# Heads' rows through DRAM, filler products on TensorE, and a new order in the first chunks and short slots

## The chip, the cores and the metric

One core of a Trainium2 chip runs the whole program. The metric is the device time of one execution in microseconds. Three runs of the kernel before gave 1003.18, 1003.45 and 1007.49 us; the median is 1003.45 us.

## The reference

A complex linear recurrence runs over 4 batches, 8 heads, 768 steps and a head width of 48; two layers of a gated network follow on its 3072 tokens.

```python
mag = np.sqrt(a_re * a_re + a_im * a_im)
scale = np.minimum(mag, 0.999) / (mag + 1e-06)           # a is scaled to this length
for t in range(S):                                       # S = 768, per batch and head, state 48 x 48
    new_re = ar * S_re - ai * S_im                       # ar, ai: [:, :, t, :, None]
    new_im = ar * S_im + ai * S_re
    S_re, S_im = new_re + einsum('bhd,bhe->bhde', k[:, :, t], v[:, :, t]), new_im
    y[:, :, t] = einsum('bhd,bhde->bhe', q[:, :, t], S_re)
x = y as (3072, 384)                                     # tokens x (heads * width)
h = x @ w_in;  x = (h * clip(h + 3, 0, 6) / 6) @ w_out              # w_in 384 x 2048
h = x @ w2_in; out = (max(h, 0) + alpha * min(h, 0)) @ w2_out
```

## The kernel before, in words

The recurrence is done in 24 chunks of 128 steps, six to a batch. For one chunk the Scalar engine (ACT) and the Vector engine (DVE) work out, from `a`, the length and angle of each step (`squares`, `logs`, `inverses`, `angle` on ACT; `mags`, `residue`, `refine`, `ratio`, `decays` on DVE), the running products and angles (`forward`, `phases`, `fractions`, `backward` on DVE), cosine and sine (`waves` on ACT), and from these the turned queries and keys (`with_qk`, `product(c, 0)`, `product(c, 1)` on DVE). The products lie in `prod` with 128 rows: rows 0 to 95 hold heads 0 to 5 in pairs, rows 96 to 127 hold the two last heads, 32 rows of their 96 in each of three columns. TensorE wants real and imaginary rows of a head stacked in 96 rows, in `st`. `stack(c)` on SyncE's queue (SP) moves them there by 12 small transfers within the on-chip memory: for each of the two products two for heads 0 to 5 (`low_stack`) and four for the last heads (`high_stack`). Where `two_queues(c)` holds (the first chunks and those made in a short slot), ACT's queue issues two of the twelve.

TensorE then makes a chunk's scores (`score`, two halves), turns its keys (`turn_k`, copied by ACT's `copy_k`), and after DVE's `mask` the outputs (`outputs`) and the new state (`new_state`, added by DVE's `state`). ACT's `x_high` and DVE's `x_low` split the outputs into a high and a low part for the layers.

The first layer runs in ten units: six of 256 columns, four of 384; the second in six units of 512. A unit has 16 items, one for each 128 of the 2048 hidden columns. Item `n` has a `hidden` product (three passes of high and low parts; one 32-bit pass in unit 0), a gate (`gate_of` on ACT, `gate1` on DVE), the split of the gated columns (`high` on ACT, `low` on GpSimd), and an `output` product. TensorE runs `hidden` three items ahead, ACT and DVE the gate two items ahead. At a unit's end ACT's `leave` empties the accumulators. ACT's and DVE's `split_w` split the first layer's weights into high and low parts, 24 blocks, one an item from item 3 on.

The order is written out by hand. `SHORT` and `LONG` cut one chunk's steps into letters, and `places()` deals them over the items of a slot: slot `s` (5 to 8 items, given by `LENGTHS`) holds TensorE's work on chunk `c0 = s`, the second half of the preparation of `c1 = s + 1`, and the first half of `c2 = s + 2`. Slots 2 to 14 are short (`is_short`: units of 256 columns), the others long. Each engine has its own loop over `places()` and runs its steps in the order of its loop; a step that waits holds all behind it on that engine. In a short slot the items' letters are `a`, `cf`, `deos`, `glv`, `hi`, `j`, `kb`. The first two chunks come ahead of item 0, in an order of their own on each engine.

In a slot's first item ACT runs `gate_of`, `copy_k(c0, 0)`, `waves(c1)`, then `high`; in its second `gate_of`, `copy_k(c0, 1)`, `logs(c2)` with a table load, `high`, `copy_ends(c1)`, the weight split and, at a unit's end, `leave`. DVE runs `phases(c1)` and `fractions(c1)` ahead of the first item's `gate1`, and `mask` behind `backward` in the second. In the third item DVE runs `gate1`, `with_qk(c1)` and `product(c1, 0)`, in the fourth `gate1` and `product(c1, 1)`. SP runs `stack(c1)` in the fourth item, `load_qk(c2)` behind it, `load_v(c1)` in the sixth and `load_a(c0 + 4)` in the last. `score(c1, 0)` waits for all twelve transfers.

Of the kernel before, what the change touches and what calls it, by code (L numbers as in the profile page):

```python
# [7 lines left out]
F32 = mybir.dt.float32  # L8
# [45 lines left out]

HIGH_PARTS = [(96, 32, 0, 6, 0), (96, 16, 1, 6, 32), (112, 16, 1, 7, 0), (96, 32, 2, 7, 16)]
STACK_DMAS = 2 * (2 + len(HIGH_PARTS))

# [20 lines left out]
B_BLOCKS = [(1, n) for n in range(NWI)]  # L78
W_ORDER = [b for q in range(NQ) for b in A_BLOCKS[q] + B_BLOCKS[(0, 1, 3, 6)[q]:(1, 3, 6, NWI)[q]]]

W_ITEM = 3
NRP = 12
# [51 lines left out]

def two_queues(c):

    return c <= FIRST or is_short(c - 1)


def splits_at(n):  # L140

    return range(max(0, n - W_ITEM), min(max(0, n + 1 - W_ITEM), len(W_ORDER)))

# [63 lines left out]
def build(nc, a_in, qk_in, v_in, w1_in, w1_out, w2_in, w2_out, alpha, x2_dram, out):  # L207
    with ExitStack() as ctx:
# [73 lines left out]
        guard = raw[0:ROWS2, 0:GUARD * 2 * PAIRS * CH].rearrange("p (c x t) -> p c x t", c=GUARD, x=2)  # L282

        hp = ctx.enter_context(nc.psum_tensor("hp", [P, 2, 512], F32))
        op = ctx.enter_context(nc.psum_tensor("op", [P, KT_DM, 512], F32))
# [9 lines left out]
        a_landed = [sem(f"a_landed{i}") for i in range(2)]  # L295
        st_landed = [sem(f"st_landed{i}") for i in range(2)]
        qk_landed, v_landed = sem("qk_landed"), sem("v_landed")
        wa_landed = [sem(f"wa_landed{i}") for i in range(10)]
# [56 lines left out]

        def high_stack(c, x):
            return [(st[x * HD + d0:x * HD + d0 + rows, c % 2, h, :, :].rearrange("p q t -> p (q t)"),
                     prod[p0:p0 + rows, x, k, :, :].rearrange("p q t -> p (q t)")) for p0, rows, k, h, d0 in HIGH_PARTS]

# [33 lines left out]
        def _(sp):  # L393
# [69 lines left out]
            load_qk(1)  # L463
            stack(0)
            load_a(3)
            load_w(7)
            stack(1)
            load_qk(2)
            load_v(1)
            for k in range(KT_DM):  # L470
                load_w(2 * k + 1)
            load_a(4)
            stack(2)
            load_w(8)
            load_w(9)
# [5 lines left out]
            for steps, n, c0, c1, c2, c3 in places():  # L481
                if "g" in steps:
                    if c1 is not None:
                        stack(c1)
                    if c2 is not None:
                        load_qk(c2)
                if "j" in steps and c1 is not None:
# [101 lines left out]
        def _(act):  # L589
# [3 lines left out]

            def logs(c):
                if c > 0:
# [26 lines left out]
            def copy_ends(c):  # L622
                act.wait_ge(end_step, 2 * c + 1)

                if c > 0:
                    act.wait_ge(st_landed[(c - 1) % 2], 16 * STACK_DMAS * ((c - 1) // 2 + 1))
                act.activation(prod[:, :, :, 0, CH], end_floor[:, c, :].unsqueeze(1).to_broadcast([P, 2, KT_DM]),
                               ACT.Copy).then_inc(ends_set, 1)

            def waves(c):  # L630
# [6 lines left out]
                               ).then_inc(trig_set, 1)  # L637

            def stack(c):
                act.wait_ge(ends_set, c + 1)  # L640
                act.wait_ge(prod_done, 2 * c + 2)
                for to, rows in low_stack(c, 1):
                    act.dma_start(to, rows).then_inc(st_landed[c % 2], 16)

# [69 lines left out]
            squares(2)  # L714
            stack(0)
            waves(1)
            copy_ends(1)
            logs(2)
            copy_k(0, 0)
            stack(1)  # L720
            inverses(2)
            copy_k(0, 1)
            x_high(0)
            angle(2)
            squares(3)
            copy_ends(2)
            copy_k(1, 0)
            waves(2)
            copy_k(1, 1)
            logs(3)  # L730
            x_high(1)
            inverses(3)
            stack(2)
            gate_of(0)
            gate_of(1)
            squares(4)
            for n in range(ALONE):
                gate_of(n + GSTEP)
                if n == 0:
                    angle(3)  # L740

            for steps, n, c0, c1, c2, c3 in places():
                keeps = not is_last(c0)
                gate_of(n + GSTEP)
                if "a" in steps:
                    if keeps:
                        copy_k(c0, 0)
                    if c1 is not None:
                        waves(c1)
                if "c" in steps:  # L750
                    if keeps:
                        copy_k(c0, 1)
                    if c2 is not None:
                        logs(c2)
                if "s" in steps and c3 is not None:
# [3 lines left out]
                if "h" in steps:  # L759
                    x_high(c0)  # L760
                    if c1 is not None and two_queues(c1):
                        stack(c1)
                if "k" in steps and c2 is not None:
                    angle(c2)
                if n + GSTEP >= MT_FF:
                    high(n + GSTEP)
                if "c" in steps and c1 is not None:
                    copy_ends(c1)
                for w in splits_at(n):
                    split_w(w)  # L770
                if n % MT_FF == MT_FF - 1:
                    leave(n // MT_FF)
            for n in range(N1 - MT_FF, NT):
# [39 lines left out]
        def _(dve):  # L813
# [69 lines left out]
            def product(c, x):  # L883
                dve.wait_ge(trig_set, c + 1)

                if c > 0:
                    dve.wait_ge(st_landed[(c - 1) % 2], 16 * STACK_DMAS * ((c - 1) // 2 + 1))
                dve.wait_ge(qb_done, c + 1)
# [125 lines left out]
            forward(1)  # L1014
            backward(1)
            phases(1)
            fractions(1)
            with_qk(1)
            mags(2)
            product(1, 0)  # L1020
# [4 lines left out]
            decay_parts(2)  # L1025
            forward(2)
            backward(2)
            phases(2)
            mask(1, 0)
            fractions(2)  # L1030
            state(0)
            mask(1, 1)
            with_qk(2)
            mags(3)
            product(2, 0)
            product(2, 1)
            residue(3)
            refine(3)
            ratio(3)
            gate1(0)  # L1040
            decays(3)
            gate1(1)
            state(1)
# [3 lines left out]
            for n in range(1, ALONE):  # L1047
                gate1(n + GSTEP)

            for steps, n, c0, c1, c2, c3 in places():  # L1050
# [10 lines left out]
                if "e" in steps and c1 is not None:  # L1061
                    product(c1, 0)
                if "f" in steps:
                    mask(c0, 0)
# [155 lines left out]
        def _(pe):  # L1220
            def score(c, k):
                if k == 0:
                    pe.wait_ge(st_landed[c % 2], 16 * STACK_DMAS * (c // 2 + 1))
                    if c >= FIRST:
# [107 lines left out]

            for c in range(FIRST):
                for k in range(2):
                    score(c, k)
                    turn_k(c, k)
                outputs(c)
                if c < FIRST - 1:
                    new_state(c)
            hidden(0)  # L1340
# [84 lines left out]
```

## Time and profile before

| | us |
|---|---|
| median of the runs | 1003.45 |
| the profiled execution | 1005.47 |
| its span | 1003.8 |
| TensorE busy | 961.2 (96%) |
| weight loads busy | 864.6 |
| DVE busy | 583.0 (58%) |
| ACT busy | 502.1 (50%) |
| GpSimd busy | 269.9 (27%) |

The profile is one execution. An engine's busy time is the sum over its instructions; the waits say which engine or transfer ended an engine's idle time; the chain of waits follows the work that ended last back from its end. Matmul ends are modelled, so a busy TensorE may still run slowly: the length of like instructions at different times tells more.

### The profile page before, as it was taken

The page shows a single profiled execution, that of the slowest core. Times are in us where ns is not written, and L with a number is a line of the kernel's source. Part 1 is how long each engine was busy: PE and PEld are TensorE (multiplying, and loading weights), DVE is VectorE, ACT ScalarE, POOL GpSimd, SP SyncE. Part 2 cuts the span into 40 slices and gives each one's busy share as a digit, 9 for nine tenths or more (in the row PEclk, how much of TensorE's full clock was granted, in tenths as well). Part 3 has the DMA queues.
Part 4 walks back from the last instruction along what each step waited for, and adds up shares of the span by engine and source line. Part 5 has one row for each costly group of instructions (what it writes and reads, how often), then busy time and mean ns, then how long its engine had stood idle before and what let it go on. Part 6 is the DMA issues. An engine that isn't in the chain of part 4 may idle for free.

```text
span 1003.8 us, 17714 instructions
## 1 busy us (share of the span) xinstructions
PE 961.2 (96%) x6786; PEld 864.6 (86%) x6786; DVE 583.0 (58%) x1049; ACT 502.1 (50%) x907; POOL 269.9 (27%) x251
## 2 busy tenths in 40 slices
PE   0899988999999999999999999999999999999998
PEld 0788988899999999999999998888888888888786
DVE  6767886867777767777662345444434444344332
ACT  7766877667877777776643443322222222222211
POOL 0000222222333322322222333332333333323232
PEclk9999999999999999999999999999999999999999
DMA  7753333332333332333320801023060060230000
GB/s 206 202 131 80 96 75 97 93 101 73 88 96 101 97 98 72 95 88 81 82 70 2 306 1 56 1 72 87 0 153 6 1 157 1 72 86 1 32 1 32
DMA packets 83589, 79.97 MB, mean 80 GB/s; under 512 B 32688, under 2 KB 78256, under 8 KB 83120
## 3 DMA queue, kind: packets, MB, share of 16 engines
q1 hardware_dynamic: 78384, 74.07, 27.7%
q10 hardware_dynamic: 5120, 4.76, 1.9%
q8 instruction: 54, 0.88, 0.4%
q14 instruction: 31, 0.25, 0.1%
HBM read 50.34 MB, written 9.44 MB: 60 GB/s over the span
## 4 chain that ended last, share of the span: by engine, by line
PE 85%; DVE 5%; ACT 3%; issue 2%; SPq 2%; DMA 1%; ACTq 0%; DVEq 0%
PE op L1262 12%; PE hp L1263 12%; PE op L1263 12%; PE hp L1262 12%; PE op L1264 12%; PE hp L1264 12%; PE yp L1250 3%; PE gp L1257 2%; PE hp L1285 2%; PE gp L1229 2%; PE yp L1229 2%; PE op L1310 2%; SPq L437 1%; PE tp L1238 1%; DMA st<-prod 1%
## 5 line engine op out<-in xcount | busy, mean ns | idle before, releaser
L572 POOL TENSOR_TENSOR g_lo<-gated,g_hi 128x512 fp32r<-128x512 f32 (+2 forms) x240 | 267.7, 1116 | 726.0 <-ACT g_hi L673 726.0
L673 ACT ACTIVATE g_hi<-gated 128x512 fp32r<-128x512 f32 (+2 forms) x240 | 126.3, 526 | 320.7 <-DVE gated L968 273.7
L964 DVE TENSOR_SCALAR gate<-hp,alpha_sb 128x512 f32<-128x512 f32 x96 | 72.0, 750 | 209.4 <-PE hp L1264 209.4
L953 DVE SCALAR_TENSOR_TENSOR gated<-gate,hp 128x256 f32<-128x256 f32 (+1 forms) x160 | 75.2, 470 | 134.2 <-ACT gate L666 133.8
L1262 PE MATMUL op<-g_hi,wb_hi 128*128 128x256 f32 (+1 forms) x432 | 137.3, 318 | 3.3 <-ACT out_sb L678 2.0
L1262 PE MATMUL hp<-x_hi,wa_hi 128*128 128x256 f32 (+1 forms) x432 | 134.7, 312 | 1.8 <-DVE gated L953 1.5
L1264 PE MATMUL op<-g_hi,wb_lo 128*128 128x256 f32 (+1 forms) x432 | 132.5, 307 | 0.0
L1263 PE MATMUL op<-g_lo,wb_hi 128*128 128x256 f32 (+1 forms) x432 | 132.3, 306 | 0.0
L1264 PE MATMUL hp<-x_hi,wa_lo 128*128 128x256 f32 (+1 forms) x432 | 132.2, 306 | 0.0
L1263 PE MATMUL hp<-x_lo,wa_hi 128*128 128x256 f32 (+1 forms) x432 | 132.2, 306 | 0.0
L666 ACT ACTIVATE gate<-hp,half 128x256 f32<-128x256 f32 (+1 forms) x160 | 81.1, 507 | 93.1 <-PE hp L1264 80.9
L1263 PE MATMUL hp<-x_lo,w2i_hi 128*128 128x512 f32 x288 | 114.6, 398 | 0.0
L1263 PE MATMUL op<-g_lo,wa_hi 128*128 128x512 f32 x288 | 113.8, 395 | 0.0
L1262 PE MATMUL hp<-x_hi,w2i_hi 128*128 128x512 f32 x288 | 113.6, 395 | 0.0
L1262 PE MATMUL op<-g_hi,wa_hi 128*128 128x512 f32 x288 | 113.6, 394 | 0.0
L1264 PE MATMUL hp<-x_hi,w2i_lo 128*128 128x512 f32 x288 | 112.9, 392 | 0.0
L1264 PE MATMUL op<-g_hi,wa_lo 128*128 128x512 f32 x288 | 112.8, 392 | 0.0
L1262 PEld LDWEIGHTS op<-g_hi,wb_hi 128*128 128x128 f32 x432 | 82.1, 190 | 5.1 <-ACT out_sb L678 2.2
L1262 PEld LDWEIGHTS hp<-x_hi,wa_hi 128*128 128x128 f32 x432 | 82.2, 190 | 2.6 <-issue 1.9
L1263 PEld LDWEIGHTS op<-g_lo,wb_hi 128*128 128x128 f32 x432 | 82.2, 190 | 0.1
L1263 PEld LDWEIGHTS hp<-x_lo,wa_hi 128*128 128x128 f32 x432 | 82.1, 190 | 0.1
L1264 PEld LDWEIGHTS op<-g_hi,wb_lo 128*128 128x128 f32 x432 | 82.1, 190 | 0.0
(113 smaller groups left out, 1645.9 us busy)
## 6 DMA issues: line engine op xcount, KB each, us to landing
st<-prod SPq DMA_DIRECT2D x64, 145.1 KB, 3.1
raw<-a_in SPq DMA_DIRECT2D x4, 2304.0 KB, 15.1
a_sb<-a_in SPq DMA_DIRECT2D x24, 288.0 KB, 3.9
qk_sb<-qk_in SPq DMA_DIRECT2D x24, 288.0 KB, 3.5
st<-prod ACTq DMA_DIRECT2D x32, 145.1 KB, 2.6
v_pad<-v_in SPq DMA_DIRECT2D x24, 192.0 KB, 3.6
x_raw<-x SPq DMA_DIRECT2D x6, 768.0 KB, 16.2
out<-out_sb SPq DMA_DIRECT2D x5, 768.0 KB, 4.2
```

The costliest lines, as they stand in the source:

```text
L572: pool.tensor_tensor(g_lo[:, at, 0:wide], gated[:, at * UT:at * UT + wide], g_hi[:, at, 0:wide].bitcast(F32), ALU.subtract).then_inc(glo_d ...
L666: act.activation(gate[:, n % 2 * UT:n % 2 * UT + wide], hp[:, n % 2, 0:wide], ACT.Relu, bias=half[:, 0:1], scale=1.0 / 6.0).then_inc(gate_ ...
L673: act.activation(g_hi[:, at, 0:wide], gated[:, at * UT:at * UT + wide], ACT.Copy).then_inc(ghi_done, 1)
L953: dve.scalar_tensor_tensor(out=gated[:, to], in0=gate[:, at], scalar=1.0, in1=hp[:, n % 2, 0:wide], op0=ALU.min, op1=ALU.mult).then_inc(ga ...
L964: dve.tensor_scalar(gate[:, at], hp[:, n % 2, 0:wide], 0.0, alpha_sb[:, m:m + 1], ALU.min, ALU.mult).then_inc(gate_done, 1)
L1229: mm = pe.matmul(score_banks[k][:, h % G4, :], st[:, c % 2, h, 1, 0:CH], st[:, c % 2, h, 0, 0:CH], start=True, stop=True)
L1250: mm = pe.matmul(y_place(c)[q * BAND:(q + 1) * BAND, j, :], weights, st[:, c % 2, h, 0, 0:CH] if of_state else scores[:, h, :], start=firs ...
L1257: mm = pe.matmul(kv_place(c)[:, h, :], k_rows[:, h, :], v_pad[:, h * PADW:h * PADW + HD], start=True, stop=True)
L1262: pe.matmul(acc, lhs[0], rhs[0], start=start, stop=False)
L1263: pe.matmul(acc, lhs[0], rhs[1], start=False, stop=False)
L1264: return pe.matmul(acc, lhs[1], rhs[0], start=False, stop=stop)
L1285: mm = pe.matmul(hp[:, n % 2, 0:wide], wa_raw[:, at], x_raw[:, u, k, 0:wide], start=k == 0, stop=k == KT_DM - 1)
```

## The change

`high_stack` goes. The 32 rows of the last two heads go out to a DRAM buffer, `rows_dram`, with one transfer for each product (`high_out`) and come back into `st` with one more each (`high_in`), which SP issues in a new step `stack_high` once the first has landed. A chunk's stack is then 8 transfers, all of SP's queue; ACT's `stack` and `two_queues` go. In a slot SP issues `load_qk(c2)` between `stack(c1)` and `stack_high(c1)`.

TensorE gets `busy(count)`: products of a tile of ones with itself into an unused bank, 36 of them among the first two chunks' steps, the first 20 as soon as `product(0, 1)` is done.

On ACT and DVE the order of the first three chunks' steps is written anew. In short slots ACT runs `high`, the weight splits and `leave` straight behind `gate_of` and `copy_k` and ahead of `waves`, `logs`, `squares`, `inverses` and `angle` (the table load of `logs` goes ahead of `high`), and DVE runs `gate1` ahead of `phases` and `fractions`, and `mask` ahead of `backward`. The weight splits follow a plan, `SPLIT_PLAN`: one or two an item from item 1 on, so that the last comes in item 16 (it was item 26).

```diff
-W_ORDER = [b for q in range(NQ) for b in A_BLOCKS[q] + B_BLOCKS[...]]
-W_ITEM = 3
+def usable(block):
+    return -(-(block[1] + 1) * WPC // DM) if block[0] else block[2] * WPC // P + 1
+def split_plan():
+    left = [b for q in range(NQ) for b in A_BLOCKS[q]] + B_BLOCKS
+    plan = {}
+    for n in range(1, 2 * MT_FF):
+        plan[n] = [b for b in left if usable(b) <= n][:1 + n % 2]
+        left = [b for b in left if b not in plan[n]]
...
+        def high_out(x):
+            return (rows_dram[x].rearrange("(k i) f -> i k f", i=HIGH),
+                    prod[LOW:P, x, :, :, :].rearrange("p k q t -> p k (q t)"))
+        def high_in(c, x):
+            return (st[x * HD:x * HD + HD, c % 2, 6:HEADS, :, :].rearrange("p h q t -> p h (q t)"),
+                    rows_dram[x].rearrange("(h d) f -> d h f", d=HD))
...
 # SP, stack(c)
-                sp.wait_ge(prod_done, 2 * c + 1)
-                for to, rows in low_stack(c, 0) + high_stack(c, 0):
-                    sp.dma_start(to, rows).then_inc(st_landed[c % 2], 16)
-                sp.wait_ge(prod_done, 2 * c + 2)
-                for to, rows in high_stack(c, 1) + ([] if two_queues(c) else low_stack(c, 1)):
+                for x in range(2):
+                    sp.wait_ge(prod_done, 2 * c + x + 1)
+                    to, rows = high_out(x)
+                    sp.dma_start(to, rows).then_inc(rows_out[x], 16)
+                    for to, rows in low_stack(c, x):
+                        sp.dma_start(to, rows).then_inc(st_landed[c % 2], 16)
+            def stack_high(c):
+                for x in range(2):
+                    sp.wait_ge(rows_out[x], 16 * (c + 1))
+                    to, rows = high_in(c, x)
                     sp.dma_start(to, rows).then_inc(st_landed[c % 2], 16)
...
 # ACT, a slot's item
+                if "a" in steps and keeps:
+                    copy_k(c0, 0)
+                if "c" in steps and keeps:
+                    copy_k(c0, 1)
+                if is_short(c0):
+                    if "c" in steps and c2 is not None:
+                        act.preload_act_table_set("natural_log_exp_and_others")
+                    behind_gate(n)                 # high(n + GSTEP), split_w, leave
+                    if "c" in steps and c1 is not None:
+                        copy_ends(c1)
+                if "a" in steps and c1 is not None:
+                    waves(c1)
+                if "c" in steps and c2 is not None:
+                    logs(c2, is_short(c0))
...
 # DVE, a slot's item
+                if is_short(c0):
+                    gate1(n + GSTEP)
                 if "a" in steps and c1 is not None:
                     phases(c1)
                     fractions(c1)
-                gate1(n + GSTEP)
+                if not is_short(c0):
+                    gate1(n + GSTEP)
+                elif "f" in steps:
+                    mask(c0, 0)
+                    mask(c0, 1)
...
 # TensorE, the first chunks
+            def busy(count):
+                for _ in range(count):
+                    pe.matmul(hp[:, 1, 0:CH], ones[:, :], ones[:, :], start=True, stop=True)
+            pe.wait_ge(consts_set, 2)
+            pe.wait_ge(prod_done, 2)
+            busy(20)
+            score(0, 0)
+            turn_k(0, 0)
+            score(0, 1)
+            busy(4)
+            turn_k(0, 1)
+            busy(3)
+            outputs(0)
+            busy(3)
+            new_state(0)
+            busy(6)
+            score(1, 0)
+            score(1, 1)
+            turn_k(1, 0)
+            outputs(1)
+            turn_k(1, 1)
```

## Rows read from the trace of the kernel before

**Rows 1.** Busy time by stretch; columns: stretch, length, each engine's busy time, clock, DMA.

```profile
26.94:47.26 20.32, 18.49 (x161) 16.63 (x161) 15.28 (x29) 15.45 (x28) 0.00 (x0) 1.00 0.82 228
47.26:98.33 51.07, 51.07 (x399) 45.46 (x400) 36.45 (x77) 34.86 (x65) 0.00 (x0) 1.00 0.42 104
98.33:203.39 105.06, 95.96 (x940) 91.81 (x939) 82.90 (x165) 77.69 (x157) 26.70 (x31) 0.98 0.36 92
203.39:1003.80 800.41, 795.69 (x5291) 710.70 (x5290) 429.74 (x733) 355.35 (x630) 241.04 (x209) 1.00 0.26 69
199.98:203.39 3.41, 3.41 (x18) 3.41 (x18) 0.83 (x2) 2.24 (x5) 0.72 (x1) 0.50 0.54 143
```

**Rows 2.** TensorE's waits from 98.33 to 203.39: total us, times, longest.

```profile
PE gp L1229 <- DMA st<-prod: 2.4, 3, 1.6
PE op L1262 <- ACT out_sb L678: 2.0, 1, 2.0
PE yp L1250 <- DVE scores L911: 1.6, 2, 0.8
PE hp L1262 <- DVE gated L953: 1.5, 1, 1.5
PE op L1262 <- POOL g_lo L572: 1.3, 3, 0.9
```

**Rows 3.** TensorE in order of time, score products of four chunks: start, length.

```profile
26.94 2.08 PE L1229 MATMUL gp<-st 96*128 96x128 f32 x8 [26.94 <-DMA st<-prod]
...
60.50 1.06 PE L1229 MATMUL gp<-st 96*128 96x128 f32 x8
...
221.17 1.06 PE L1229 MATMUL gp<-st 96*128 96x128 f32 x8
...
242.21 1.05 PE L1229 MATMUL gp<-st 96*128 96x128 f32 x8
```

**Rows 4.** The chain of waits, from chunk 1's last transfer to its outputs.

```profile
35.32 2.48 DMA st<-prod
...
43.11 3.58 PE op L1250 x64
```

**Rows 5.** The chain of waits in slot 7: start, length, what.

```profile
182.29 1.28 ACT L596
...
187.21 1.28 DVE prod L889
...
194.51 3.92 DMA st<-prod
```

**Rows 6.** ACT in order of time, last item of slot 8, first of slot 9.

```profile
219.70 1.28 ACT L616 ACT_TABLE_LOAD   x1
...
221.98 0.40 ACT L673 ACTIVATE g_hi<-gated 128x256 fp32r<-128x256 f32 x1
222.29 0.45 ACT L666 ACTIVATE gate<-hp,half 128x256 f32<-128x256 f32 x1
```

**Rows 7.** DVE in order of time, same place and slot 9.

```profile
219.93 0.41 DVE L953 SCALAR_TENSOR_TENSOR gated<-gate,hp 128x256 f32<-128x256 f32 x1
...
222.23 1.67 DVE L845 TENSOR_TENSOR_SCAN t_phase<-ones,t_frac,t_dt 128x128 f32<-128x128 f32 x3
...
232.35 1.27 DVE L889 TENSOR_TENSOR prod<-t_fb,t_trig 128x768 f32<-128x768 f32 x1
```

**Rows 8.** SP's issues in slot 9: start, time to issue, lines, transfers.

```profile
233.71 4.10 SPq L437 DMA_DIRECT2D st<-prod  x6
237.85 2.48 SPq L440 DMA_DIRECT2D st<-prod  x4
240.38 0.61 SPq L399 DMA_DIRECT2D qk_sb<-qk_in  x1
241.03 1.07 SPq L403 DMA_DIRECT2D qk_sb<-qk_in  x2
```

**Rows 9.** Transfers by size over the span: KB each, median us from issue to landing.

```profile
st<-prod SPq DMA_DIRECT2D x64, 145.1 KB, 3.1
...
x<-out_sb SPq DMA_DIRECT2D x2, 192.0 KB, 3.5
```

**Rows 10.** DVE's weight splits by form: busy, mean ns.

```profile
L905 DVE TENSOR_TENSOR wb_lo<-wb_raw,wb_hi 128x512 fp32r<-128x512 f32 x12 | 8.6, 717 | 6.4 <-ACT wb_hi L683 6.4
```

More of the change, by code:

```diff
@@ L53 @@
 TW = CH + 1
[L55 to L56 removed]
+ROWS_DMAS = 2 * 3
 N1 = U1 * MT_FF
@@ L78 @@
 B_BLOCKS = [(1, n) for n in range(NWI)]
-W_ORDER = [b for q in range(NQ) for b in A_BLOCKS[q] + B_BLOCKS[(0, 1, 3, 6)[q]:(1, 3, 6, NWI)[q]]]
-W_ITEM = 3
+def usable(block):
[6 more added lines that the diff above has]
+        left = [b for b in left if b not in plan[n]]
+    assert not left
+    return plan
+SPLIT_PLAN = split_plan()
+W_ORDER = [b for n in SPLIT_PLAN for b in SPLIT_PLAN[n]]
 NRP = 12
@@ L132, in is_short @@
     return width(items_of(s)[-1] // MT_FF) == FIRST * CH
-def two_queues(c):
-    return c <= FIRST or is_short(c - 1)
 def splits_at(n):
-    return range(max(0, n - W_ITEM), min(max(0, n + 1 - W_ITEM), len(W_ORDER)))
+    return [W_ORDER.index(b) for b in SPLIT_PLAN.get(n, [])]
 def split_count(blocks):
@@ L282, in build @@
         guard = raw[0:ROWS2, 0:GUARD * 2 * PAIRS * CH].rearrange("p (c x t) -> p c x t", c=GUARD, x=2)
+        rows_dram = nc.dram_tensor("rows", (2, LOW, 2 * TW), F32, kind="Internal").ap()
         hp = ctx.enter_context(nc.psum_tensor("hp", [P, 2, 512], F32))
@@ L296, in build @@
         st_landed = [sem(f"st_landed{i}") for i in range(2)]
+        rows_out = [sem(f"rows_out{i}") for i in range(2)]
         qk_landed, v_landed = sem("qk_landed"), sem("v_landed")
@@ L486, in _ @@
                         load_qk(c2)
+                    if c1 is not None:
+                        stack_high(c1)
                 if "j" in steps and c1 is not None:
@@ L592, in squares, with logs @@
                 act.activation(t_sq[:, :, :, :], a_sb[:, c % 2, :, :, :], ACT.Square).then_inc(squares_set, 1)
-            def logs(c):
-                if c > 0:
+            def logs(c, loaded=False):
+                if c > 0 and not loaded:
                     act.preload_act_table_set("natural_log_exp_and_others")
@@ L637, in waves @@
                                ).then_inc(trig_set, 1)
[L639 to L643, printed above, removed]
             def copy_k(c, k):
@@ L719, in _, with behind_gate @@
             copy_k(0, 0)
-            stack(1)
             inverses(2)
+            x_high(0)
             copy_k(0, 1)
-            x_high(0)
             angle(2)
             squares(3)
+            waves(2)
+            copy_k(1, 0)
             copy_ends(2)
-            copy_k(1, 0)
-            waves(2)
+            x_high(1)
             copy_k(1, 1)
             logs(3)
-            x_high(1)
+            gate_of(0)
             inverses(3)
-            stack(2)
-            gate_of(0)
             gate_of(1)
             squares(4)
+            def behind_gate(n):
+                if n + GSTEP >= MT_FF:
+                    high(n + GSTEP)
+                for w in splits_at(n):
+                    split_w(w)
+                if n % MT_FF == MT_FF - 1:
+                    leave(n // MT_FF)
             for n in range(ALONE):
                 gate_of(n + GSTEP)
+                for w in splits_at(n):
+                    split_w(w)
                 if n == 0:
@@ L744, in _ @@
                 gate_of(n + GSTEP)
[L745 to L754, printed above, removed]
+                if "a" in steps and keeps:
[12 more added lines that the diff above has]
+                    logs(c2, is_short(c0))
                 if "s" in steps and c3 is not None:
@@ L760, in _ @@
                     x_high(c0)
-                    if c1 is not None and two_queues(c1):
-                        stack(c1)
                 if "k" in steps and c2 is not None:
                     angle(c2)
[L765 to L772, printed above, removed]
+                if not is_short(c0):
+                    if n + GSTEP >= MT_FF:
+                        high(n + GSTEP)
+                    if "c" in steps and c1 is not None:
+                        copy_ends(c1)
+                    if n % MT_FF == MT_FF - 1:
+                        leave(n // MT_FF)
             for n in range(N1 - MT_FF, NT):
@@ L1014, in _ @@
             forward(1)
-            backward(1)
             phases(1)
             fractions(1)
+            mags(2)
+            backward(1)
             with_qk(1)
-            mags(2)
             product(1, 0)
@@ L1026, in _ @@
             forward(2)
-            backward(2)
[L1028 to L1032, printed above, removed]
+            state(0)
+            phases(2)
+            fractions(2)
+            mask(1, 0)
+            mask(1, 1)
+            backward(2)
             with_qk(2)
-            mags(3)
             product(2, 0)
             product(2, 1)
+            mags(3)
+            gate1(0)
             residue(3)
@@ L1039, in _ @@
             ratio(3)
-            gate1(0)
+            gate1(1)
             decays(3)
-            gate1(1)
             state(1)
@@ L1048, in _ @@
                 gate1(n + GSTEP)
+                for w in splits_at(n):
+                    split_w(w)
             for steps, n, c0, c1, c2, c3 in places():
+                if is_short(c0):
+                    gate1(n + GSTEP)
                 if "a" in steps and c1 is not None:
@@ L1062, in _ @@
                     product(c1, 0)
-                if "f" in steps:
+                if "f" in steps and not is_short(c0):
                     mask(c0, 0)
@@ L1331, in second_half @@
                     hidden(n + HSTEP)
[L1333 to L1339, printed above, removed]
+            def busy(count):
[19 more added lines that the diff above has]
+            turn_k(1, 1)
             hidden(0)
```

16 lines of the change are left out of this document (8 added, 8 removed).

## The prediction, made before the changed kernel ran

> **What bounds the kernel now.** I read four views in this order: busy time by stretch, TensorE's waits, the chain of waits, and the single instructions of a few slots. The stretches are to be read first, because the 96% of the span hides three stages [rows 1]. From 203.39 us on, TensorE is busy for 795.69 of 800.41 us and the rest is the tail; from 47.26 to 98.33 it never idles. In these two stages only fewer products would help, and the change removes none. What can move lies in the other two. Up to 47.26 the first two chunks go through all engines one after the other. From 98.33 to 203.39 TensorE idles 105.06 - 95.96 = 9.1 us, and for 3.41 us it ran at a granted clock of 0.50, the lower of its two levels (1.2 and 2.4 GHz), which cost half of that, 1.7 us [rows 1]; the fall came right behind a wait of 1.6 us for a stack transfer [rows 2]. So at most about 10.8 us are to be had there. The waits tell whose they are [rows 2]: 2.4 us on the stacks, 2.0 on `leave`, 1.6 on the masks, 2.8 on the gate and on g_lo.
>
> In the first stage the durations tell the clock: eight score products take 2.08 us at 26.94 and 1.06 at 60.50 [rows 3], so the first chunks run at the lower level, although the clock column reads 1.00 there [rows 1].
>
> The chain in slot 7 shows what makes a stack late [rows 5]: ACT's table load for `logs`, then the gate, DVE's product, SP's issues one after the other, and a last transfer from 194.51 to 198.43. Whatever is put ahead of these steps on ACT or DVE, and each transfer on SP, reaches TensorE when the next score comes.
>
> **The first chunks.** Chunk 0's stack landed at 26.9. After: products end where they did, at 18.9; SP issues six transfers of 0.65 us (ten took 6.58 [rows 8]), from 18.8 to 22.7; the second `high_in` must wait for its `high_out`, issued at 20.7 and landed 3.1 to 3.5 later [rows 9], and lands itself near 26.5. This stack gains 0.4 us at most. Chunk 1's lands at 35.32 + 2.48 = 37.80 [rows 4]; with six issues for ten ahead of it and SP free earlier I get 36.7.
>
> From there the clock decides. Chunk 1 now needs 47.26 - 37.80 = 9.5 us: scores, masks, outputs (3.58 us [rows 4]), the copy of the outputs. At the higher level the products halve: scores 0.9 + 0.9 us, the last mask 0.7, outputs 1.9, copy 0.6, together 5.0, and `hidden(0)` starts at 36.7 + 5.0 = 41.7, a gain of 5.5. If the clock rises only with the dense run of chunk 0's products, near 35, the path is `copy_k`, `angle(2)` and `phases(2)`, now ahead of chunk 1's masks on DVE, to 40.5, then masks, outputs and copy, 44.4: a gain of 2.8. If it stays low through both chunks, the 16 fillers behind `busy(20)`, 0.23 us each at that level (2.08 / 9, one product's length being drain [rows 3]), stand partly on the path, and `hidden(0)` comes at 48.7, a loss of 1.5. I take the middle of the two gains, 4.2. Unit 0 then runs as before, only earlier: its weights and chunk 2's stack have several us of slack.
>
> On this the Trainium skill speaks against the change (TensorE: Matmul & The Clock Gate, "HAM oscillation — how this bites in real kernels"): a wait for a transfer between bursts of products sets the clock back, and each burst begins slowly again. `busy(20)` ends near 23.4 and the first score waits until 26.5, so by that rule the 20 fillers would buy nothing. That a fall can follow a shorter wait the row at 0.50 shows [rows 1]. It is the third rival below.
>
> **Short slots: what goes.** Gate, high part and `leave` now stand ahead of the table functions on ACT, `gate1` ahead of the scans on DVE, and masks ahead of `backward`. The waits of TensorE for masks, gate, g_lo and `leave`, 1.6 + 1.5 + 1.3 + 2.0 = 6.4 us [rows 2], should go but for one place: the last item of slot 3 has `high`, two splits and `leave` ahead of `angle`, some 2.4 us, and slot 4's second gate comes about 1.4 us too late for `hidden`. The splits, 24 at 0.7 us on DVE [rows 10] and a like time on ACT, end ten items earlier. Ten of them leave slots 4 and 5 for unit 0, where DVE is busy 36.45 of 51.07 us [rows 1], so they cost nothing there.
>
> **Short slots: what comes.** The same steps now stand ahead of the chain that makes the next stack. In the last item of a slot, `angle`'s table load began at 219.70, right behind the gate [rows 6]. It now waits for `gate1`, which ended at 220.34 [rows 7], and for `high`, 0.40 us [rows 6]: 1.0 us later. `phases` began at 222.23 as soon as the angle was there [rows 7]; now the first item's `gate_of` and `gate1`, 0.45 + 0.41 us [rows 6, 7], are ahead of it, so 1.7 later. Of this, 0.4 comes back, since `high` no longer stands between `waves` and the second item's gate. `product(c1, 0)` ended at 232.35 + 1.27 = 233.62, 12.45 us after its slot's start at 221.17 [rows 3, 7]; I take 13.6, bounds 13.0 and 14.2.
>
> From there to the landing: before, ten issues, 4.10 + 2.48 [rows 8], and the last landing about 2 us behind its issue, some 8.0 us in all. After: six stack issues (4.0), `load_qk` in between (0.61 + 1.07 and the gaps, 1.75 [rows 8]), two `high_in` (1.3). The last is issued 6.4 us after the product and lands 2.2 to 3.1 later, 2.5 taken: near the 3.1 of the 145 KB stack transfers [rows 9], being 99 KB. That makes 8.9, bounds 8.6 and 9.5. The wait for `rows_out` is hidden: a store of 192 KB to DRAM takes 3.5 us [rows 9], and the second one has 4.3. Without `load_qk` as cover it would not be. The skill (DMA: Bandwidth & Descriptors, "Anatomy of one DMA — SWDGE (gpsimd) path") puts most of a transfer's fixed 2 us into the receipt of the write and calls HBM the heaviest target; by it the round trip is an estimated 4 us, by the rows up to 6.6.
>
> So a stack lands 13.6 + 8.9 = 22.5 us after the work of the last slot is done, and a slot of seven items is 242.21 - 221.17 = 21.04 us of TensorE's work [rows 3]. If a slot begins `s` us late for lack of its stack, ACT and DVE get those `s` us for free, so the next wait is 22.5 - 21.04 - s: 1.46 us in every other slot. A batch's last chunk has no turned keys and no new state (18.9 us of TensorE, landing 22.05), its first a cheaper output (20.1). Slot by slot, with the 0.8 us of a `leave` where one falls ahead of the chain (slots 6 and 13): 1.5 inside slot 4, then waits at the starts of slots 5 to 14 of 1.6, 1.55, 1.65, 0, 1.46, 0, 1.46, 0, 0.4, 1.8. The sum is 11.4 us in place of 10.8, a loss of 0.6.
>
> In long slots SP's 8 issues with `load_qk` end no later than the 12 did, and TensorE waits for one stack there, 0.2 us, which I take as gained.
>
> **Sum.** -4.2 + 0.6 - 0.2 = -3.8 us against the profiled 1005.47 (span 1003.8). That execution is 2.0 us above the median of the runs, and the same difference on the median gives 999.6; I forecast 999.5.
>
> **Rivals.** First, the stacks come in time: the product ends at 12.8 and lands 8.2 later, 21.0, so that TensorE waits only inside slot 4 and at slots 5 and 6, about 3 us. For it: the issues are two fewer on SP, and before the change the steady slots, 9 and 10, ran without a wait. Against it: rows 6 and 7, by which the chain is longer. It gives 999.5 - 8.4 = 991.
>
> Second, and slower than before: the stack's round trip sets the period of all short slots. If it lands at 24.2 after the slot's work (14.2 + 10.0, `high_in` queued behind the load of q and k), the waits average (24.2 - 21.04) / 2 = 1.6 in eleven slots, 17.4 for 10.8, +6.6; with 2.8 gained in front it is 1003.45 + 3.8 = 1007. It begins to lose when the stack lands later than about 23.7. For it: a stack transfer did take 3.92 us once [rows 5]. Against: the median 3.1.
>
> Third, the fillers don't hold the clock: +1.5 in front, +0.6 - 0.2, 1005.4.
>
> **Chances.** Forecast 0.44 (its own range 996 to 1003), stacks in time 0.28, round trip 0.12, low clock 0.11, others 0.05. A measurement of this kernel tells 0.5%, 5.0 us, from no change. Faster than 998.4: all of the second case and a third of the first, 0.43. Slower than 1008.5: a third of the round trip, and a part of the others, 0.08. Within: 0.49. The range 989 to 1006 leaves out the best end of the second case and the worse half of the round trip.
>
> **What would show it.** Right: eight scores of chunk 0 or 1 near 1.06 us, `hidden(0)` between 41 and 45, no waits on g_lo and masks from 98 to 203, waits of 1 to 2 us on the stack transfer in every other short slot, `product(c1, 0)` ending about 13.6 after its slot's start. Wrong: scores still at 2.08 in chunk 1; short slots of 21.04 without a wait; a stack that lands over 10 us behind its product; or a wait between 47 and 98, where I count none.

## The result, and the profile after

The changed kernel took 1021.69 us (median of four runs, 1021.56 to 1023.12), the kernel before 1004.78 beside it: a ratio of 1.0176, 95% interval 1.0158 to 1.0193. It is 1.8% slower, 17 us; the forecast was 999.5 and the range ended at 1006.

The spans of the two profiled executions differ by 1019.8 - 1003.8 = 16.0 us. Three stretches make that up. Busy time by stretch, the changed kernel; the columns are those of [rows 1]:

```profile
41.72:98.33 56.61, 53.50 (x405) 46.33 (x405) 44.85 (x91) 43.57 (x81) 0.00 (x0) 1.00 0.53 135
...
104.14:365.75 261.61, 240.87 (x2456) 230.71 (x2455) 196.92 (x365) 179.96 (x361) 70.17 (x79) 0.99 0.37 93
...
365.75:1019.80 654.05, 649.42 (x3730) 567.02 (x3729) 320.10 (x513) 245.94 (x411) 197.52 (x160) 1.00 0.24 66
247.50:250.90 3.40, 3.40 (x20) 3.40 (x19) 2.56 (x8) 2.53 (x6) 0.67 (x2) 0.50 0.35 107
```

The same stretch of the kernel before, from slot 4's first score to slot 15's:

```profile
105.93:349.98 244.05, 235.16 (x2456) 229.31 (x2455) 187.59 (x379) 183.36 (x372) 69.34 (x80) 0.99 0.35 90
```

Slot 4 began at 104.14 in place of 105.93, 1.79 us sooner. From there to slot 15, eleven short slots, the same 2456 products took 261.61 in place of 244.05 us: 17.56 more. The long slots took 654.05 for 653.82. And -1.79 + 17.56 + 0.23 = 16.0. So everything was lost in the short slots. The clock has no part in it: it fell once in each kernel, for 3.4 us. Of the 17.56 us, 20.74 - 8.89 = 11.85 are more idle time of TensorE; in the other 5.7 it counts as busy with the same products: most of that is in the first products behind a wait (27 in place of 10), each of which adds some 0.38 us to the busy time, where one in a dense run adds 0.12.

TensorE's waits in those slots (total us, times, longest), changed kernel; compare [rows 2]:

```profile
PE gp L1270 <- DMA st<-rows: 11.8, 9, 2.4
PE hp L1303 <- DVE gated L986: 7.3, 15, 1.2
PE op L1303 <- ACT out_sb L702: 1.0, 1, 1.0
PE tp L1279 <- ACT k_rows L672: 0.5, 1, 0.5
```

The waits on masks and g_lo are gone, as forecast. The waits on stacks are 11.8 us. That the forecast had 11.4 is chance, since it spread them otherwise and had nothing beside them. But `hidden` waits for `gate1` 15 times, and it was `gate1` that should have come sooner. ACT's own waits, 94 to 370 us, say why:

```profile
ACT g_hi L697 <- DVE gated L986: 58.7, 61, 1.6
ACT t_trig L663 <- DVE t_frac L888: 22.6, 11, 2.2
ACT gate L690 <- PE hp L1305: 2.3, 2, 2.0
```

Before, over 94 to 355 us:

```profile
ACT gate L666 <- PE hp L1264: 20.5, 26, 2.4
ACT t_trig L633 <- DVE t_frac L855: 18.6, 11, 3.2
ACT g_hi L673 <- DVE gated L953: 10.8, 17, 1.3
```

Before, ACT's longest waits were for TensorE, so it had time to spare. After, it stands still 61 times, about a microsecond each, because `high` is the next instruction behind `gate_of` and needs what DVE's `gate1` makes of that gate. It waits for TensorE almost never: it is behind. DVE in turn waits for ACT alone (changed kernel, 94 to 370 us):

```profile
DVE gated L986 <- ACT gate L690: 51.4, 46, 1.9
DVE x_lo L950 <- ACT x_hi L679: 9.8, 12, 0.9
```

The chain of waits at the start of slot 9 (first score at 221.69) shows one round of it; compare [rows 6, 7]:

```profile
220.10 0.48 DVE t_log L854
...
221.22 0.85 issue
222.08 0.42 DVE gated L986
...
222.52 0.42 ACT g_hi L697
222.96 1.28 ACT L646
...
225.24 0.47 ACT gate L690
...
226.06 1.68 DVE t_phase L878 x3
```

ACT's gate was done at 220.94, but DVE was in `decays` (`t_log` to `t_dt`), so `gate1` came at 222.08, `high` at 222.52 and `angle`'s table load only at 222.96. That is 1.27 us after the slot's start; in the kernel before it was 1.47 before it (219.70 against 221.17). DVE's phase scan stood behind the next `gate1`, which waited 0.77 us for a gate that ACT could only do behind `angle`.

There is one more thing on DVE. Its scans in the short slots by line (busy, mean ns), 104 to 345 us, changed kernel:

```profile
L894 DVE TENSOR_TENSOR_SCAN t_fb<-t_dt,ones 128x128 f32<-128x128 f32 x33 | 17.0, 568 | 0.4
L906 DVE TENSOR_TENSOR_SCAN t_fb<-t_dt,t_fb,ones 128x127 f32<-128x127 f32 x30 | 16.6, 606 | 0.0
L878 DVE TENSOR_TENSOR_SCAN t_phase<-ones,t_frac,t_dt 128x128 f32<-128x128 f32 x27 | 15.0, 610 | 0.0
```

and in the kernel before:

```profile
L845 DVE TENSOR_TENSOR_SCAN t_phase<-ones,t_frac,t_dt 128x128 f32<-128x128 f32 x27 | 13.6, 559 | 0.0
L873 DVE TENSOR_TENSOR_SCAN t_fb<-t_dt,t_fb,ones 128x127 f32<-128x127 f32 x33 | 13.5, 462 | 0.0
L861 DVE TENSOR_TENSOR_SCAN t_fb<-t_dt,ones 128x128 f32<-128x128 f32 x33 | 12.2, 424 | 0.4
```

The first two groups got longer by a third, the last by a tenth. E13 below is about this.

### The profile page after: what moved, and what is told of

Its sections match the earlier page's. It is cut to its first block, busy times and chain, and to the rows that moved or that the text cites. A ratio compares the mean times of both kernels' runs of the same rounds, so it can differ in the third digit from the quotient of the medians.

```text
span 1019.8 us, 17747 instructions
## 1 busy us (share of the span) xinstructions
PE 970.0 (95%) x6858; PEld 868.3 (85%) x6858; DVE 599.5 (59%) x1049; ACT 502.7 (49%) x907; POOL 271.0 (27%) x251
## 4 chain that ended last, share of the span: by engine, by line
PE 67%; ACT 13%; DVE 9%; issue 7%; SPq 2%; DMA 2%; POOL 0%; DVEq 0%; ACTq 0%
PE op L1303 10%; PE op L1304 10%; PE op L1305 10%; PE hp L1304 10%; PE hp L1303 10%; PE hp L1305 10%; ACT gate L690 2%; DVE t_phase L878 2%; DVE gated L986 2%; PE yp L1291 2%; ACT L646 2%; ACT g_hi L697 1%; PE gp L1298 1%; DMA a_sb<-a_in 1%; DVE t_fb L914 1%
```

## The experiments

"After" is the changed kernel, and ratios are to the kernel before, run beside each. Theory O says the new order on ACT and DVE costs the time, theory R the stacks' way through DRAM.

**E1, ACT's order undone.** ACT's order in short slots as before; all else as changed.

```diff
-                if is_short(c0):                    # ACT's front order
+                if False:
...
-                if not is_short(c0):
-                    if n + GSTEP >= MT_FF:
-                        high(n + GSTEP)
...
+                if n + GSTEP >= MT_FF:
+                    high(n + GSTEP)
...
```

> Changed kernel with ACT's order in the short slots put back (high, copy_ends, weight splits and leave behind the table functions); all else as changed. Theory O (order): with high straight behind gate_of, ACT stands still in each item until DVE's gate1 is done, and angle, waves and logs, which make the next stack, come that much later; so undoing it takes away most of TensorE's waits on the stacks (11.8 us) and on the gate (7.3 us): 1003 to 1008 us, and ACT's waits of high for gate1 fall from some 60 to under 20 us. Theory R (round trip): the stacks come late because their rows go through DRAM; then only the gate's waits go, 1013 to 1016 us, and the waits on the stacks stay at 10 us or more.

1004.47 us, ratio 1.0007 (0.9989 to 1.0025). With ACT's old order 17 us are back.

**E2, DVE's order undone.** `gate1` behind the scans and `mask` behind `backward` again; ACT's front order stays.

```diff
-                if is_short(c0):
-                    gate1(n + GSTEP)
...
-                if not is_short(c0):
-                    gate1(n + GSTEP)
-                elif "f" in steps:
-                    mask(c0, 0)
-                    mask(c0, 1)
+                gate1(n + GSTEP)
...
-                if "f" in steps and not is_short(c0):
+                if "f" in steps:
```

> Changed kernel with DVE's order in the short slots put back (gate1 behind phases and fractions, mask behind backward), ACT's order as changed. Theory O: the chain loses gate1's 0.9 us between angle and phases, but ACT's high then waits behind the scans, so 1016 to 1022 us. Theory R: no change within 1 us of 1021.7, since the stacks' time from product to landing stays.

1018.13 us, 1.0142 (1.0116 to 1.0168): 3.6 us less than the changed kernel.

**E3, stacks within the on-chip memory.** From chunk 3 on the twelve transfers of before, two of them issued by ACT; the new orders stay.

```diff
-                        stack(c1)
+                        stack_within(c1)       # SP: low_stack + high_stack, as before
...
-                        stack_high(c1)
...
+                    if c1 is not None and two_queues(c1):
+                        stack(c1)              # ACT: low_stack(c1, 1)
```

> Changed kernel, but from chunk 3 on the stacks go within the on-chip memory again by twelve transfers, two of them on ACT's queue in short slots (the first three chunks still go through DRAM). Product to landing falls by about 1.1 us. Theory R: the stacks' waits go almost wholly, 1008 to 1012 us. Theory O: a stack that lands 1.1 us earlier gives back half of that in each of eleven slots, since a late slot gives ACT and DVE time, 1014 to 1018 us.

1024.99 us, 1.0208 (1.0181 to 1.0235): slower still, and outside what either theory gave. TensorE's waits, 94 to 370 us:

```profile
PE hp L1336 <- DVE gated L1019: 16.2, 22, 1.8
PE gp L1303 <- DMA st<-prod: 4.0, 6, 1.9
```

The waits on stacks fell from 11.8 to 4.0 us and came back, and more, as waits on the gate (16.2 us for 7.3). ACT issues two transfers more in a slot:

```profile
242.77 0.59 ACTq L698 DMA_DIRECT2D st<-prod  x1
...
243.39 0.69 ACTq L698 DMA_DIRECT2D st<-prod  x1
```

Its next instruction started 0.1 us behind the second issue and some 0.7 us behind its last computation, in nearly every slot. That ACT, late as it is, has no time for this is the likely reason; no run took these two issues away alone. In any case a wait on a stack is not a measure of what the stack costs.

**E5, both orders undone** (E1 and E2 together).

> Changed kernel with both ACT's and DVE's orders in the short slots put back; what is left of the change is the first chunks' order with the fillers, the splits in front and the rows through DRAM. Theory O: the first chunks' gain of about 4 us shows, the slots run as before but for a stack 1 us later: 997 to 1003 us. Theory R: 1011 to 1016 us.

999.49 us, 0.9958 (0.9940 to 0.9976). What is left of the change gains 4 us, and DVE's order costs 5 with ACT's old order (1004.47 against 999.49). That this kernel takes what was forecast for another, 999.5, is chance. TensorE's waits, 94 to 370 us:

```profile
PE gp L1265 <- DMA st<-rows: 2.9, 5, 0.8
PE op L1298 <- ACT out_sb L702: 1.2, 1, 1.2
PE op L1298 <- POOL g_lo L602: 0.9, 1, 0.9
PE yp L1286 <- DVE scores L945: 0.8, 1, 0.8
PE hp L1298 <- DVE x_lo L951: 0.5, 1, 0.5
```

**E6, `high` alone moved back** behind the table functions; splits, copies and `leave` stay in front.

```diff
             def behind_gate(n):
-                if n + GSTEP >= MT_FF:
-                    high(n + GSTEP)
...
                     angle(c2)
+                if n + GSTEP >= MT_FF:
+                    high(n + GSTEP)
                 if not is_short(c0):
-                    if n + GSTEP >= MT_FF:
-                        high(n + GSTEP)
```

> Changed kernel, in which only high goes back behind the table functions in ACT's short slots; splits, leave, the table load and all of DVE's order stay in front. Theory O, in its narrow form: it is high's wait for gate1, a handshake from ACT to DVE and back in each item, that holds the table functions; so 1003 to 1009 us, and ACT's waits of high for gate1 fall from 58.7 us to under 20. Rival: it is the whole block in front (leave, splits, the early table load); then over 1014 us.

1004.06 us, 1.0005 (0.9994 to 1.0017). One instruction an item makes the same 17 us as all of ACT's order. Its ACT waits, 94 to 370 us:

```profile
ACT gate L690 <- PE hp L1303: 29.8, 32, 2.1
...
ACT g_hi L697 <- DVE gated L984: 7.5, 16, 1.2
```

ACT is ahead again, and waits for TensorE.

**E7, no fillers.** E5 without the calls of `busy`.

```diff
-            busy(20)
             score(0, 0)
...
-            busy(4)
...
```

> Both orders of the short slots put back (999.5 us), and the 36 filler products taken out. If the fillers raise the clock for the first chunks, it is slower without them: first score products at 2 us again, hidden(0) some 2 to 4 us later than 41.7, 1001 to 1004 us. If the new order of the first chunks makes the gain alone, 999 to 1000 us.

1001.24 us, 0.9981 (0.9971 to 0.9992), 1.7 us above E5. TensorE in order of time: chunk 0's scores, chunk 1's, `hidden(0)`:

```profile
25.95 2.05 PE L1265 MATMUL gp<-st 96*128 96x128 f32 x8 [25.95 <-DMA st<-rows]
...
36.78 2.04 PE L1265 MATMUL gp<-st 96*128 96x128 f32 x8
...
45.56 2.64 PE L1321 MATMUL hp<-x_raw,wa_raw 128*128 128x256 f32 x11
```

and in the changed kernel, with the fillers in front:

```profile
19.15 6.16 PE L1377 MATMUL hp<-ones 128*128 128x128 f32 x40 [19.15 <-DVE prod L922]
25.61 1.16 PE L1270 MATMUL gp<-st 96*128 96x128 f32 x8 [0.30 <-DMA st<-rows]
...
36.31 1.16 PE L1270 MATMUL gp<-st 96*128 96x128 f32 x8
...
41.72 2.86 PE L1326 MATMUL hp<-x_raw,wa_raw 128*128 128x256 f32 x12
```

Without fillers both chunks run at the lower level (2.05 us for eight scores; 2.08 before), with them at the higher. E5's `hidden(0)` starts at 42.26, so they are worth 3.3 us there and some 2 us at the end.

**E8, stacks within the on-chip memory, old orders** (E3's edit on E5).

> Both orders of the short slots put back, and from chunk 3 on the stacks by twelve transfers within the on-chip memory, two of them on ACT's queue. If the way through DRAM costs time (a stack 1 us later), the 2.9 us of waits on stacks go: 996 to 998.5 us. If it is free or better, since ACT issues nothing and SP four less, 999 to 1001 us.

997.13 us, 0.9946 (0.9933 to 0.9959). With the old orders the way through DRAM seems to cost some 1 to 2 us; the intervals of E5 and E8 overlap, so this isn't clear of the noise.

**E9, the old plan of the weight splits** in E5.

```diff
-SPLIT_PLAN = split_plan()
+W_ITEM = 3                                   # one block an item, from item 3 to 26
...
```

> Both orders of the short slots put back, and the weight splits as before, one an item from item 3 to 26. If the splits in front take load off slots 4 and 5, it is slower without: waits on gate, masks and g_lo return there, 1001 to 1004 us. If they are free where they were, 999 to 1000 us.

1003.10 us, 1.0005 (0.9994 to 1.0015): the splits in front gain some 4 us.

**E10 and E11, the parts of DVE's order.** E8 with the masks alone ahead of `backward` (E10), or `gate1` alone ahead of the scans (E11).

```diff
+                if is_short(c0) and "f" in steps:        # E10
+                    mask(c0, 0)
+                    mask(c0, 1)
...
+                if is_short(c0):                         # E11, ahead of phases
+                    gate1(n + GSTEP)
```

> E8's kernel (both orders undone, stacks within the on-chip memory from chunk 3 on; 997.13 us, 0.9946 of the kernel before) with DVE's masks alone ahead of `backward` in short slots, gate1 where it was. Theory M (DVE's front order costs by its gate1; masks in front are harmless, since they are short and their scores are there early): TensorE's waits on scores (0.8 us) go, the rest stays: 996 to 997, ratio 0.993 to 0.995. Rival N (the masks, which wait for TensorE's scores and bias half a slot's work, hold `backward` and so the next stack): waits on the stack transfers go up by 3 to 5 us, 1000 to 1002, ratio 0.997 to 0.999.

> E8's kernel with DVE's gate1 alone ahead of the scans in short slots, masks where they were. Theory M: gate1 waits for ACT's gate, which in the first item of a slot stands behind the angle and copies, so the scans and with them the stack start later; 1000 to 1002, ratio 0.997 to 0.999, with waits of TensorE on the stack transfers of 5 us or more in place of 1.8. Rival N: gate1 in front costs nothing: 996.5 to 997.5, ratio 0.994 to 0.995.

E10 took 996.09 us, 0.9925 (0.9911 to 0.9939), the fastest kernel of all. E11 took 999.71, 0.9956 (0.9942 to 0.9969). The waits on masks went with the masks in front, and with `gate1` in front the stacks came later; TensorE's waits of E10 (first two) and E11, 94 to 360 us:

```profile
PE gp L1301 <- DMA st<-prod: 1.3, 3, 0.6
PE hp L1334 <- DVE x_lo L984: 1.3, 1, 1.3
```

```profile
PE gp L1301 <- DMA st<-prod: 2.9, 4, 1.4
PE op L1334 <- POOL g_lo L627: 1.8, 2, 1.4
```

In the profiled executions slots 4 to 14 took 237.96 us in E8, 236.32 in E10 and 240.30 in E11. So of the two parts it is `gate1` that costs. E11 is clearly slower than E10 but not than E8, whose interval it overlaps, and it lies between M and N: M's waits of 5 us didn't come, and its ratio is below M's 0.997 to 0.999.

**E12, two steps more on E10**: `gate1(1)` ahead of the residue of chunk 3 (the expectation calls it chunk 2's), and `high` and `leave` ahead of the table functions in a unit's last item alone.

```diff
+            gate1(1)
             residue(3)
...
-            gate1(1)
...
+                at_end = is_short(c0) and n % MT_FF == MT_FF - 1
+                if at_end:
+                    high(n + GSTEP)
+                    leave(n // MT_FF)
```

> E10's kernel and two more steps: DVE's gate1 of item 1 ahead of chunk 2's residue in the first chunks, and in the last item of a unit alone, in short slots, ACT's high part and `leave` ahead of `waves` and `logs`. By the waits left in E8 (hidden products on gate1 between 46 and 54 us, 2.6 us; `leave` 1.3; g_lo 1.0) it gains 2 to 4 us: 993 to 995, ratio 0.990 to 0.993. Rival: what E6 showed of `high` in front (it waits for DVE) costs here too, in some seven items, 1 us each, and the gain in unit 0 is taken by a later stack of chunk 2 or 3: 997 to 1001, ratio 0.994 to 0.998.

1001.18 us, 0.9966 (0.9955 to 0.9977). The rival was right: the wait on `leave` went, but ACT's waits of `high` on `gate1` rose from 8.2 to 12.7 us, and stacks and low parts came later. Of some 5 us against E10, 0.86 are lost by chunk 2's first score (58.37 against 57.51), the rest behind it, in the short slots, where the second step acts. The waits in unit 0 stayed too, so that `gate1(1)` stood behind `residue` was not their cause.

**E13, GpSimd writes zeros.** The changed kernel, with `low` a write of zeros in the units of 256 columns, so that the low parts are missing from the products there.

```diff
             def low(n):
...
+                if wide == 256:
+                    pool.memset(g_lo[:, at, 0:wide].bitcast(F32), 0.0).then_inc(glo_done, 1)
+                    return
```

> The changed kernel, with GpSimd writing zeros into g_lo in place of gated - g_hi in the units of 256 columns (so those low parts are left out of the result). What is open: in the changed kernel DVE's scans take 55.8 us from 104 to 345 us, and 28.3 us of that lies beside GpSimd's subtraction; with `high` back (E6) they take 43.6 us and 1.0 us. One of the three scans of `forward` takes 886 ns in each slot in place of 407. Theory P (most of what `high` in front costs is this: it starts GpSimd's subtraction in the middle of DVE's scans, and the two hold each other up): with writes alone, which read nothing, the scans go back to 407 to 465 ns each, some 44 us in all, a slot's period falls by 1.1 to 1.3 us, and the time is 1007 to 1011. Theory H (ACT's standing still behind DVE's gate is the cost by itself): the scans go back but the period stays near 23.5, the time is 1018 to 1022. If zeros hold the scans up as well, the scans stay near 55 us and the run says nothing on either.

1011.68 us, 1.0078 (1.0052 to 1.0105): 10.0 us less than the changed kernel. That is 0.7 above theory P's range and far below theory H's; a slot's period fell by 0.99 us. DVE's scans, 104 to 345 us:

```profile
L909 DVE TENSOR_TENSOR_SCAN t_fb<-t_dt,t_fb,ones 128x127 f32<-128x127 f32 x33 | 13.4, 461 | 0.0
L897 DVE TENSOR_TENSOR_SCAN t_fb<-t_dt,ones 128x128 f32<-128x128 f32 x33 | 11.6, 407 | 0.4
L881 DVE TENSOR_TENSOR_SCAN t_phase<-ones,t_frac,t_dt 128x128 f32<-128x128 f32 x27 | 11.1, 465 | 0.0
```

They are at their short length again, though ACT still waits 48.6 us, 61 times, for `gate1`. In the changed kernel one of `forward`'s three scans took 877 to 898 ns in every slot and the others 392 to 425; GpSimd's subtraction lies over the first of them and into the second, which is the long one (GpSimd's spans are rough). Of the three scans in `phases` and in `backward` one was as long in nearly every slot. So `high` in front costs in two ways: it starts GpSimd's subtraction in the middle of DVE's scans, which holds them up; and ACT stands still. The run puts up to 10 of the 17 us on the first. It is an upper end, because the zeros also shorten a `prod` and `t_dt` that were slowed in E6 too (`t_dt` 933 ns in E6, 558 here), and are written in 0.32 us. A long scan is not enough for the loss either: in E5 one of `phases` was long in most slots.

## Why the prediction was wrong

**The step that failed** is this one: "If a slot begins `s` us late for lack of its stack, ACT and DVE get those `s` us for free, so the next wait is 22.5 - 21.04 - s: 1.46 us in every other slot." The table gives, for the ten stacks made in slots 5 to 14, the mean from a slot's first score to the end of `product(c1, 0)`, from there to the landing, and the mean distance of the slots' first scores (nine distances; in slot 9 of the changed kernel: 221.69, 237.15, 246.64 and the next score at 246.68).

| kernel | product | landing | sum | slot's period |
|---|---|---|---|---|
| before | 12.89 | 8.51 | 21.40 | 21.91 |
| after | 14.10 | 9.25 | 23.35 | 23.53 |
| E2 | 13.84 | 9.14 | 22.98 | 23.04 |
| E13 | 13.17 | 9.16 | 22.33 | 22.54 |
| E6 | 12.75 | 9.31 | 22.06 | 22.21 |
| E1 | 12.23 | 9.29 | 21.52 | 21.79 |
| E5 | 11.95 | 9.16 | 21.11 | 21.22 |

The period is the chain, to 0.1 to 0.3 us, in every kernel with stacks through DRAM. In the changed kernel nearly every slot begins when its stack lands, and the next chain takes its full length from there. Nothing is given back. By the forecast's own 22.5 the eleven slots would then have lost 11 x (22.5 - 21.91) = 6.5 us against before, not 0.6; with the measured period it is 11 x (23.53 - 21.91) = 17.8, near the 17.56 of the same trace.

The table alone doesn't say which engine sets the period, since chain and period must agree wherever TensorE waits for its stack. The waits do. The step takes it that ACT and DVE have time to spare when TensorE is late. In the changed kernel, from 104.14 to 365.75 us, ACT was busy for 179.96 us and waited 57.3 + 22.6 us for DVE, together 259.9 of 261.61; the profile lists no wait of ACT for TensorE there, and DVE's waits are for ACT. So the round of ACT and DVE, 23.6 us a slot, is longer than TensorE's 21.04 by itself, and a slot that begins late gives it nothing. The forecast has no term for this round. In E1, E5 and E6, with `high` back, ACT waits 33 to 40 us for TensorE over the same slots, and the period falls to 21.2 to 22.2 us.

**The chain's length** was the second miss. The forecast's 13.6 was put on slot 9's own 12.45, a slot that had not waited; the mean before was 12.89. Its rise of 1.15 us was right in size (1.21 measured), but by luck: the cause was not the sum of 1.0 and 0.7 that it gave, and in slot 9 itself the rise was 3.0 us (15.46). There the table load came 2.74 us later against the slot's start (1.27 + 1.47), not 1.0, since `gate1` stood behind `decays`; what E6 and E13 take away was not thought of at all. The costs of `gate1` and `high` were taken as their own durations, and the forecast looked for their waits in two items where they come in all.

**The landing**: 8.9 forecast, 9.25 measured, inside 8.6 to 9.5. The profile has the two legs apart (KB each, median us from issue to landing):

```profile
st<-prod SPq DMA_DIRECT2D x96, 145.1 KB, 3.1
...
rows<-prod SPq DMA_DIRECT2D x48, 96.8 KB, 2.3
st<-rows SPq DMA_DIRECT2D x48, 96.8 KB, 2.9
```

The estimate of about 4 us for the round trip, by "Anatomy of one DMA — SWDGE (gpsimd) path" in the Trainium skill's DMA: Bandwidth & Descriptors, is below the 5.2 of these rows; that section is on transfers issued by GpSimd, and these are SP's. Most of the 5.2 us lies beside SP's other issues: from product to landing E5 takes 9.16 us and E8 8.62.

**The first chunks** came as the first of the three cases: scores at 1.16 us, chunk 0's stack at 25.6 (26.5 forecast), chunk 1's at 36.3 (36.7), `hidden(0)` at 41.72 (41.7). The middle of 4.2 was too careful there, and too high further on: of 5.5 us, 3.65 were left at chunk 2's scores (56.85 against 60.50) and 1.79 at slot 4. "A wait between 47 and 98, where I count none" came: `hidden` on `gate1`, and 1.9 us on `x_lo`. The `x_lo` wait is 0.5 us in E1, E5, E8 and E11, 1.3 in E2 and E10, 1.9 in E6. What makes it, and the `gate1` wait in unit 0, stays open.

**The splits** cost nothing, as forecast, but gained some 4 us (E9), which was not in the sum as a term of its own: the forecast asked what the earlier splits would hold up, and not what the old ones held up in the ten items behind.

**The rivals.** "Stacks in time" is what E5 is: its chain of 21.11 us fits the 21.04, and it gives 999.5, not 991, since in the old order the waits on `leave`, g_lo and masks are back, and the stacks still cost 2.9 us. The round trip "sets the period" was right in that every slot was late, and put the point of loss at a landing 23.7 after the slot's work; but 23.35 already cost 17 us, as the price was halved by the same rule, and E3 shows that the round trip isn't the cause. The third, fillers that don't hold the clock, is refuted by E7. Its premise, and that of the 16 fillers at 0.23 us, was an error of count: a filler is two products in the trace (40 for 20), so `busy(20)` ended at 25.3 and the first score waited 0.30 us, not 3. The rule of the Trainium skill (TensorE: Matmul & The Clock Gate, "HAM oscillation — how this bites in real kernels") was thus not put to the test here. Elsewhere the trace agrees in part: the clock fell to 0.50 at 247.50, 0.8 us behind a stack wait of 1.6 us, but not behind those of 2.4 and 2.1 us at slots 13 and 14.

## What to carry to other kernels

Before moving a step ahead of others on an in-order engine, look at what it waits for: a short instruction whose input comes back from a second engine holds the whole queue for the round trip, in every item, and the price is the wait and not its duration. Where two engines wait for each other, add up one engine's work and its waits for the other over a slot: if that is more than the third engine's work, it is the slot's period, and a late start of the third engine gives nothing back. And look at what a step that comes earlier sets going on yet another engine.

## What the runs showed of the hardware

A scan on DVE that reads two tensors of the on-chip memory (128 x 128) took 0.39 to 0.48 us by itself. In the changed kernel it took up to 0.90 us while GpSimd subtracted two tensors (in E5 once 1.23); in E13, where GpSimd wrote zeros beside it, 0.40 to 0.47. The Trainium skill (GPSIMD Engine Reference, "1. Specifications") says that the two engines share their interfaces to that memory, with contention where DVE's instruction has two inputs there; these rows agree, and show that writes alone did not disturb the scans.

The granted clock's column read 1.00 while like products took about twice as long, 2.05 us in E7 against 1.16 in the changed kernel, as in [rows 1, 3]: at the start of the program the lengths tell the clock and the column does not. Two issues of a transfer took 0.59 and 0.69 us on ACT's queue in E3, and held ACT's next instruction up by some 0.7 us together.
